# Later pairs' attention in eight groups, one TensorE burst per layer step

## The chip, the cores and the metric

The kernel runs on one core of one Trainium2 chip. The metric is device time in microseconds of one execution; lower is better.

## What is computed

Attention at two scales over four batches of eight heads (576 tokens, head width 64), then two feed-forward layers over the 2304 tokens of width 512, inner width 2048. All in fp32.

```python
# down-sampled: means over 4 tokens, softmax attention over 144, repeated 4 times
out_d = sm_attn(q_d, k_d, v_d)
out_up = np.repeat(out_d, 4, axis=2)
# local: only keys with |i - j| < 4
scores = np.where(mask, scale * q @ k.T, -1e9)
attn = softmax(scores)
x = out_up + attn @ v
...
h = x @ w_in;  g = np.maximum(0.01 * h, h);  x = g @ w_out      # layer 1
h = x @ w_in;  g = h - np.tanh(h);           out = g @ w_out    # layer 2
```

## The kernel before

Two heads make a *pair*; there are 16 pairs. Attention of one pair is cut into 17 *steps* (`STEPS`), and every engine has an `attention(step, ...)` that does its share: steps 0 to 3 turn q and k with the tensor engine (TensorE) and copy them out on ScalarE, step 4 computes the local scores, step 6 the down-sampled ones, steps 5 to 10 are the softmax (VectorE maximum, shift and sums; ScalarE exponentials; GpSimd the products with the inverse sums, `pl` at L993 and `pd` at L998), 11 to 14 turn the probabilities (L391, L396), 15 and 16 multiply by v. Two PSUM banks are shared by the steps and handed over by semaphores (`bank_full`, `bank_free`).

The first four pairs run alone (`batch0`). Then layer 1 runs in 8 tiles of 288 tokens. The first six (`MIXED`) are *mixed*: between their matmuls stand the steps of two later pairs each. Within a tile, f runs over the 16 blocks of the inner width (`CF`). At each f, TensorE does `hidden1(f)`, called H(f) below, 12 matmuls into the PSUM bank `ph1[f % 2]`, and `down1(f - 2)`, called D(f - 2), 12 matmuls into `acc`. Every product of fp32 numbers is split in a high part (rounded to fp32r) and a low part (the difference), three matmuls a product. Between H(f) and D stand these elementwise operations:

- ScalarE: `leak`, 0.01 h into `g1` (L684); VectorE: the maximum of leak and h (L887); ScalarE: the rounding `g_hi` (L664, in `split_g`); VectorE: `g_lo` (L872, in `lo_of_g1`).
- For f from 8 on, weights are split as they come: ScalarE `in_hi` (L648) and `out_hi` (L652), GpSimd `in_lo` (L1009) and `out_lo` (L1014).
- `next_x` (`ahead`) splits the next tile's x: `x_hi` (L657), `x_lo` (L867). The next tile's H(0) runs before D(15) of this one. `keep_y` copies the finished `acc` back.

The order is written out by hand, engine by engine. Slot 2f stands behind H(f) and slot 2f + 1 behind D(f - 2); a function `later` gives the step of a slot, four ahead (`HEAD`), since `batch0` has done the first four of pair 4's steps:

```python
def later(slot, tile):
    return (slot + HEAD) % STEPS, A, 2 * tile + 2 + (slot + HEAD) // STEPS
```

ScalarE rounds g_hi(f - 1) behind leak(f); `next_x` and `out_hi(15)` stand ahead of g_hi(15).

Of the kernel before, what the change touches and what calls it, by code (L numbers as in the profile page):

```python
# [24 lines left out]
ALU = mybir.AluOpType  # L25
# [14 lines left out]
HEAD = 4  # L40
KEPT_SLOTS = (20, 25)
# [16 lines left out]
def two_scale_attention_and_feed_forward(nc, q, k, v, w_in1, w_out1, w_in2, w_out2, out):  # L58
# [36 lines left out]
    with ExitStack() as ctx:  # L95
# [146 lines left out]
        def later(slot, tile):  # L242

            return (slot + HEAD) % STEPS, A, 2 * tile + 2 + (slot + HEAD) // STEPS
# [116 lines left out]
        def _(pe):  # L361
# [117 lines left out]
            def hidden1(tile, f):  # L479
# [7 lines left out]
                wait_from(pe, g_done, n - 1)  # L487
# [22 lines left out]
            def layer1(tile, between, begun=True, ahead=True):  # L510
                for f in range(CF + LAG1):
                    if f < CF and not (begun and f == 0):
                        hidden1(tile, f)
                    between(2 * f)
# [4 lines left out]
                    between(2 * f + 1)  # L519
# [44 lines left out]
            def mixed(tile, slots=2 * STEPS, begun=True):  # L564
                def between(slot):
                    if slot < slots:
                        attention(*later(slot, tile))
                layer1(tile, between, begun)

            def nothing(slot):  # L570
                pass

# [5 lines left out]
            mixed(0, begun=False)  # L578
            with pe.Fori(1, MIXED - 1) as tile:
                mixed(tile)  # L580
            mixed(MIXED - 1, 2 * STEPS - HEAD)
            for tile in range(MIXED, TILES1):
                layer1(tile, nothing, ahead=tile < TILES1 - 1)
# [7 lines left out]
        def _(act):  # L591
# [80 lines left out]
            def layer1(tile, between, extra, keep_before, ahead):  # L672
# [28 lines left out]
            def mixed(tile, keep_before, slots=2 * STEPS):  # L701
                def between(slot):
                    if slot < slots:
                        attention(*later(slot, tile))
                layer1(tile, between, nothing, keep_before, lambda: next_x(tile + 1))
# [94 lines left out]
        def _(dve):  # L800
# [79 lines left out]
            def layer1(tile, between, extra, keep_before, ahead):  # L880
                for f in range(CF + 1):
                    n = CF * tile + f
                    if f == CF:
                        ahead()
# [230 lines left out]
```

## Time and profile before

| | us |
|---|---|
| median of three runs | 989.72 |
| lowest and highest | 986.1, 992.62 |
| profiled execution, whole | 990.84 |
| its span | 989.1 |
| TensorE busy in it | 956.0 |
| mean granted TensorE clock | 0.984 |

The profile is of one execution on the one core. Times in its rows are from the span's start. In the rows, PE is TensorE's matmuls, PEld its weight loads, DVE VectorE, ACT ScalarE, POOL GpSimd, SP SyncE; PEclk is the granted share of the tensor clock, 1.00 being 2.4 GHz and 0.50 being 1.2 GHz.

### The profile page before, as it was taken

How to read it: one execution, taken by the hardware profiler on the slowest of the kernel's cores; microseconds unless marked ns; L12 is line 12 of the kernel's file. 1: busy time of each engine (PE TensorE's matmuls, PEld its weight loads, DVE VectorE, ACT ScalarE, POOL GpSimd, SP SyncE). 2: the span in 40 equal slices, each digit the busy share in tenths (PEclk: the TensorE clock that was granted, in tenths of full speed). 3: DMA queues.
4: the chain of work that ended last, by engine and by line, in shares of the span. 5: the costliest groups of instructions: out<-in, count | busy, mean ns of one | idle time of the engine just before them, and what ended most of it. 6: DMA issues, size and time to landing. Idle time of an engine off the chain costs nothing.

```text
span 989.1 us, 19759 instructions
## 1 busy us (share of the span) xinstructions
PE 956.0 (97%) x6960; PEld 892.1 (90%) x6960; DVE 579.4 (59%) x1066; ACT 554.5 (56%) x1355; POOL 411.5 (42%) x341
## 2 busy tenths in 40 slices
PE   6789999999999999999999999999999999999998
PEld 5678999999999999999999988889899899898996
DVE  5745653664556446635324766776676676766764
ACT  4445644544635446446354767775575666766654
POOL 4535732723616417227161837623233233233232
PEclk9769999999999999999999999999999999999999
DMA  7842421022112211210100302100000000000000
GB/s 168 179 138 66 112 50 35 16 49 49 25 24 49 49 25 24 49 27 10 55 1 30 110 24 76 42 33 1 1 32 1 32 0 0 32 0 0 32 1 32
DMA packets 87797, 41.48 MB, mean 42 GB/s; under 512 B 60352, under 2 KB 81344, under 8 KB 87744
## 3 DMA queue, kind: packets, MB, share of 16 engines
q1 hardware_dynamic: 87744, 40.78, 15.7%
q8 instruction: 33, 0.54, 0.2%
q14 instruction: 20, 0.16, 0.1%
HBM read 36.04 MB, written 4.72 MB: 41 GB/s over the span
## 4 chain that ended last, share of the span: by engine, by line
PE 78%; ACT 6%; DVE 6%; POOL 5%; issue 3%; DMA 2%; SPq 0%; ACTq 0%; POOLq 0%; DVEq 0%
PE ph L474 12%; PE ph L476 11%; PE ph L475 11%; PE acc L550 6%; PE acc L551 6%; PE acc L552 6%; PE acc L503 6%; PE acc L504 5%; PE acc L505 5%; PE banks L372 3%; PE banks L404 2%; DVE g_lo L872 2%; POOL pl L993 2%; PE banks L391 2%; POOL g_lo L1039 1%
## 5 line engine op out<-in xcount | busy, mean ns | idle before, releaser
L1039 POOL TENSOR_TENSOR g_lo<-scratch,g_hi 128x384 fp32r<-128x384 f32 x96 | 126.1, 1314 | 259.3 <-ACT g_hi L664 259.3
L887 DVE TENSOR_TENSOR g<-g,ph 128x288 f32<-128x288 f32 x128 | 57.9, 452 | 189.4 <-ACT g L684 188.5
L1009 POOL TENSOR_TENSOR in_lo<-w_whole,in_hi 128x512 fp32r<-128x512 f32 x64 | 83.8, 1310 | 160.9 <-ACT in_hi L648 159.7
L474 PE MATMUL ph<-x_hi,w_hi_a 128*128 128x288 f32 (+1 forms) x448 | 144.7, 323 | 1.9 <-DVE x_lo L867 1.9
L684 ACT ACTIVATE g<-ph 128x288 f32<-128x288 f32 x128 | 52.5, 410 | 157.2 <-PE ph L476 155.8
L476 PE MATMUL ph<-x_hi,w_lo_a 128*128 128x288 f32 (+1 forms) x448 | 140.5, 314 | 0.0
L475 PE MATMUL ph<-x_lo,w_hi_a 128*128 128x288 f32 (+1 forms) x448 | 140.4, 313 | 0.0
L923 DVE SCALAR_TENSOR_TENSOR scratch<-scratch,ph 128x384 f32<-128x384 f32 x96 | 53.2, 554 | 112.9 <-ACT scratch L729 108.0
L1014 POOL TENSOR_TENSOR out_lo<-w_whole,out_hi 128x512 fp32r<-128x512 f32 x64 | 86.4, 1350 | 56.3 <-ACT out_hi L652 55.6
L728 ACT ACTIVATE scratch<-ph 128x384 f32<-128x384 f32 x96 | 46.8, 488 | 108.4 <-PE ph L476 106.8
L872 DVE TENSOR_TENSOR g_lo<-g,g_hi 128x288 fp32r<-128x288 f32 x128 | 88.6, 692 | 2.7 <-ACT g_hi L664 2.7
L474 PEld LDWEIGHTS ph<-x_hi,w_hi_a 128*128 128x128 f32 x448 | 84.9, 189 | 5.2 <-issue 3.1
L475 PEld LDWEIGHTS ph<-x_lo,w_hi_a 128*128 128x128 f32 x448 | 84.9, 190 | 1.4
L476 PEld LDWEIGHTS ph<-x_hi,w_lo_a 128*128 128x128 f32 x448 | 84.9, 189 | 0.0
L503 PE MATMUL acc<-g_hi,out_hi 128*128 128x288 f32 x256 | 79.1, 309 | 2.5 <-DVE g_lo L872 2.5
L503 PE MATMUL acc<-g_hi,w_hi_a 128*128 128x288 f32 x256 | 78.7, 307 | 1.9 <-DVE g_lo L872 1.9
L474 PE MATMUL ph<-x_hi,in_hi 128*128 128x288 f32 x256 | 78.8, 308 | 0.0
L504 PE MATMUL acc<-g_lo,w_hi_a 128*128 128x288 f32 x256 | 76.0, 297 | 0.0
L505 PE MATMUL acc<-g_hi,w_lo_a 128*128 128x288 f32 x256 | 75.9, 296 | 0.0
L505 PE MATMUL acc<-g_hi,out_lo 128*128 128x288 f32 x256 | 75.6, 295 | 0.0
L475 PE MATMUL ph<-x_lo,in_hi 128*128 128x288 f32 x256 | 75.6, 295 | 0.0
L504 PE MATMUL acc<-g_lo,out_hi 128*128 128x288 f32 x256 | 75.5, 295 | 0.0
(162 smaller groups left out, 2688.8 us busy)
## 6 DMA issues: line engine op xcount, KB each, us to landing
out_dram<-o_stage SPq DMA_DIRECT2D x18, 256.0 KB, 2.0
w_whole<-in_moe_w_in_dram SPq DMA_DIRECT2D x16, 256.0 KB, 3.6
w_whole<-in_moe_w_out_dram SPq DMA_DIRECT2D x16, 256.0 KB, 4.4
qn<-in_q_dram SPq DMA_DIRECT2D x28, 144.0 KB
kn<-in_k_dram SPq DMA_DIRECT2D x28, 144.0 KB
v4n<-in_v_dram SPq DMA_DIRECT2D x28, 144.0 KB
vw<-in_v_dram SPq DMA_DIRECT2D x28, 122.5 KB
scratch<-in_moe_w_in_dram SPq DMA_DIRECT2D x8, 256.0 KB, 2.9
```

The source lines that it names most:

```text
L474: pe.matmul(bank, whi, x_hi[:, c, 0:width], start=(c == 0), stop=False)
L475: pe.matmul(bank, whi, x_lo[:, c, 0:width], start=False, stop=False)
L476: last = pe.matmul(bank, wlo, x_hi[:, c, 0:width], start=False, stop=(c == CD - 1))
L503: pe.matmul(acc[:, c, 0:T1], whi, g1_hi[:, f % 3, :], start=(f == 0), stop=False)
L504: pe.matmul(acc[:, c, 0:T1], whi, g1_lo[:, f % 3, :], start=False, stop=False)
L505: last = pe.matmul(acc[:, c, 0:T1], wlo, g1_hi[:, f % 3, :], start=False, stop=(f == CF - 1))
L550: pe.matmul(acc[:, j, 0:DM], hi, whi, start=(f == 0), stop=False)
L551: pe.matmul(acc[:, j, 0:DM], hi, wlo, start=False, stop=False)
L872: dve.tensor_tensor(g1_lo[:, f % 3, :], g1[:, f % 2, :], g1_hi[:, f % 3, :].bitcast(F32), ALU.subtract).then_inc(g_lo_done, 1)
L1009: pool.tensor_tensor(in_lo[:, f % 2, :], w_whole[:, f - KEPT, 0:DM], in_hi[:, f % 2, :].bitcast(F32), ALU.subtract).then_inc(in_lo_done, 1)
L1014: pool.tensor_tensor(out_lo[:, f % 2, :], w_whole[:, f - KEPT, DM:CW], out_hi[:, f % 2, :].bitcast(F32), ALU.subtract).then_inc(out_lo_don ...
L1039: pool.tensor_tensor(g2_lo[:, f % 3, :], g2[:, f % 2, :], g2_hi[:, f % 3, :].bitcast(F32), ALU.subtract).then_inc(g_lo_done, 1)
```

## The change

The steps are taken in eight groups (`GROUPS`), one group at each f, and all of TensorE's part of a group runs as one burst behind D(f - 2). The last two f of a tile take groups 0 and 1 of the pair after (`GROUP_HEAD`). VectorE's local maximum and shift move from step 6 into step 5 and so stand in the scores' group. The maximum is written into the PSUM bank in place, and g_hi and g_lo read it there; so ScalarE rounds g_hi(f) at the same f as its leak, and H(f) waits for `g_lo_done` of f - 2, not `g_done`. `next_x` stands at f = 15 right behind g_hi(15) and g_lo(15). `split_in(f + 2)` stands right behind leak(f), and `split_out(f)` at the end of f.

```diff
+GROUPS = ((0, 1), (2, 3), (4, 5), (6, 7, 8), (9, 10), (11, 12), (13, 14), (15, 16))
+GROUP_HEAD = 2
-        def later(slot, tile):
-            return (slot + HEAD) % STEPS, A, 2 * tile + 2 + (slot + HEAD) // STEPS
+        def later(f, tile, last):
+            if f < last:
+                pair, group = divmod(f + GROUP_HEAD, len(GROUPS))
+                for step in GROUPS[group]:
+                    yield step, A, 2 * tile + 2 + pair
...
 # TensorE, hidden1
-                wait_from(pe, g_done, n - 1)
+                wait_from(pe, g_lo_done, n - 1)
...
 # TensorE, layer1
                     if f < CF and not (begun and f == 0):
                         hidden1(tile, f)
-                    between(2 * f)
                     if ahead and f == CF + LAG1 - 1:
                         hidden1(tile + 1, 0)
                     if f >= LAG1:
                         down1(tile, f - LAG1)
-                    between(2 * f + 1)
+                    for step, s, i in later(f, tile, last):
+                        attention(step, s, i)
...
 # ScalarE, layer1
-                    if f == CF:
-                        ahead()
-                    if f - 1 >= KEPT:
-                        split_out(tile, f - 1)
                     if f < CF:
                         act.wait_ge(h_done, n + 1)
-                        wait_from(act, g_lo_done, n - 1)
+                        wait_from(act, g_done, n - 1)
                         act.activation(g1[:, f % 2, :], ph1[:, f % 2, 0:T1], ACT.Copy, scale=0.01)\
                             .then_inc(leak_done, 1)
                     if f == 0:
                         keep_before()
-                    if f:
-                        split_g(n - 1, f - 1, g1[:, (f - 1) % 2, :], g1_hi)
-                    between(2 * f)
                     if KEPT <= f + 2 < CF:
                         split_in(tile, f + 2)
+                    if f < CF:
+                        split_g(n, f, ph1[:, f % 2, 0:T1], g1_hi)
+                    if f == CF - 1:
+                        ahead()
+                    for step, s, i in later(f, tile, last):
+                        attention(step, s, i)
                     extra(f)
-                    between(2 * f + 1)
+                    if KEPT <= f < CF:
+                        split_out(tile, f)
...
 # VectorE
-                elif step == 6:
                     dve.wait_ge(s.bank_free[1], uses1(i, 3))
                     dve.tensor_reduce(s.mxl[:, :], s.pl[:, :, :], AX_X, ALU.max).then_inc(s.max_l, 1)
...
-                dve.tensor_tensor(g1_lo[:, f % 3, :], g1[:, f % 2, :], g1_hi[:, f % 3, :].bitcast(F32),
+                dve.tensor_tensor(g1_lo[:, f % 3, :], ph1[:, f % 2, 0:T1], g1_hi[:, f % 3, :].bitcast(F32),
                                   ALU.subtract).then_inc(g_lo_done, 1)
...
-                        dve.tensor_tensor(g1[:, f % 2, :], g1[:, f % 2, :], ph1[:, f % 2, 0:T1], ALU.max)\
+                        dve.tensor_tensor(ph1[:, f % 2, 0:T1], g1[:, f % 2, :], ph1[:, f % 2, 0:T1], ALU.max)\
                             .then_inc(g_done, 1)
...
 # GpSimd, layer1
-                    if f - 1 >= KEPT:
-                        split_out(tile, f - 1)
-                    between(2 * f)
                     if KEPT <= f + 2 < CF:
                         split_in(tile, f + 2)
-                    between(2 * f + 1)
+                    for step, s, i in later(f, tile, last):
+                        attention(step, s, i)
+                    if KEPT <= f:
+                        split_out(tile, f)
```

What this makes of the order is shown at two places, both in the second pair of a mixed tile, f = 9 to 11. On ScalarE, before, from leak(9) on (L684 leak, L664 g_hi, L648 in_hi, L652 out_hi, L607 the local exponential, L611 the down-sampled ones, L616 a copy of turned probabilities):

```order
301 L684 ACTIVATE g<-ph 128x288
302 L664 ACTIVATE g_hi<-g 128x288
303 L648 ACTIVATE in_hi<-w_whole 128x512
304 L652 ACTIVATE out_hi<-w_whole 128x512
305 L684 ACTIVATE g<-ph 128x288
306 L664 ACTIVATE g_hi<-g 128x288
307 L607 ACTIVATE pl<-pl 128x630
308 L648 ACTIVATE in_hi<-w_whole 128x512
309 L611 ACTIVATE pd,rs<-banks,mxd 96x144 x3
310 L652 ACTIVATE out_hi<-w_whole 128x512
311 L684 ACTIVATE g<-ph 128x288
```

and after, from leak(9) on (L676 leak, L660 g_hi, L644 in_hi, L648 out_hi, L603 and L607 the exponentials):

```order
302 L676 ACTIVATE g<-ph 128x288
303 L644 ACTIVATE in_hi<-w_whole 128x512
304 L660 ACTIVATE g_hi<-ph 128x288
305 L603 ACTIVATE pl<-pl 128x630
306 L607 ACTIVATE pd,rs<-banks,mxd 96x144 x3
307 L648 ACTIVATE out_hi<-w_whole 128x512
308 L676 ACTIVATE g<-ph 128x288
309 L644 ACTIVATE in_hi<-w_whole 128x512
310 L660 ACTIVATE g_hi<-ph 128x288
```

The exponentials stood at f = 10 around in_hi(12); now they stand at f = 9, ahead of out_hi(9), and leak(10) and in_hi(12) come behind them.

On GpSimd, before, at the same place (L986 the value sums `vd`, L1009 in_lo, L1014 out_lo, L993 the norm of the local probabilities, L998 that of the down-sampled ones):

```order
110 L1014 TENSOR_TENSOR out_lo<-w_whole,out_hi 128x512
111 L1009 TENSOR_TENSOR in_lo<-w_whole,in_hi 128x512
112 L1014 TENSOR_TENSOR out_lo<-w_whole,out_hi 128x512
113 L993 TENSOR_TENSOR pl<-pl,rs 128x630
114 L1009 TENSOR_TENSOR in_lo<-w_whole,in_hi 128x512
115 L998 TENSOR_TENSOR pd<-pd,rs 96x432
116 L1014 TENSOR_TENSOR out_lo<-w_whole,out_hi 128x512
```

and after (L997 in_lo, L1002 out_lo, L981 and L986 the norms):

```order
108 L997 TENSOR_TENSOR in_lo<-w_whole,in_hi 128x512
109 L1002 TENSOR_TENSOR out_lo<-w_whole,out_hi 128x512
110 L997 TENSOR_TENSOR in_lo<-w_whole,in_hi 128x512
111 L981 TENSOR_TENSOR pl<-pl,rs 128x630
112 L986 TENSOR_TENSOR pd<-pd,rs 96x432
113 L1002 TENSOR_TENSOR out_lo<-w_whole,out_hi 128x512
114 L997 TENSOR_TENSOR in_lo<-w_whole,in_hi 128x512
```

The local norm came behind out_lo(10) and ahead of in_lo(13); now it comes one block earlier, behind in_lo(12).

On TensorE the local probabilities were turned in two bursts of four with D(10) between them, the first behind H(12). Now they are turned in one burst behind D(9) (L508 to L510 down1, L396 the turning, L479 and L480 hidden1):

```order
1217 L508 MATMUL acc<-g_hi,out_hi 128x288
1218 L509 MATMUL acc<-g_lo,out_hi 128x288
1219 L510 MATMUL acc<-g_hi,out_lo 128x288
1220 L396 MATMUL banks<-ident,pl 70x128 x8
1221 L479 MATMUL ph<-x_hi,in_hi 128x288
1222 L480 MATMUL ph<-x_lo,in_hi 128x288
```

where before stood

```order
1242 L475 MATMUL ph<-x_lo,in_hi 128x288
1243 L476 MATMUL ph<-x_hi,in_lo 128x288
1244 L391 MATMUL banks<-ident,pl 70x128 x4
1245 L503 MATMUL acc<-g_hi,out_hi 128x288
1246 L504 MATMUL acc<-g_lo,out_hi 128x288
```

## Rows read from the trace of the kernel before

**Rows 1.** The page: busy time of TensorE, its share of the span, matmuls

```profile
PE 956.0 (97%) x6960; PEld 892.1 (90%) x6960; DVE 579.4 (59%) x1066; ACT 554.5 (56%) x1355; POOL 411.5 (42%) x341
```

**Rows 2.** Two stages: length, busy of PE, PEld, DVE, ACT, POOL, then PEclk, DMA

```profile
272.20:339.80 67.60, 66.75 (x618) 64.12 (x618) 35.97 (x70) 33.44 (x89) 29.76 (x27) 1.00 0.16 36
...
468.50:577.00 108.50, 107.42 (x803) 106.60 (x802) 52.64 (x90) 56.41 (x124) 46.84 (x33) 1.00 0.15 47
```

**Rows 3.** Waits of TensorE from 137 to 577 us, all there are

```profile
PE banks L391 <- POOL pl L993: 2.7, 10, 0.3
PE acc L503 <- DVE g_lo L872: 2.5, 7, 0.8
```

**Rows 4.** Timeline of TensorE around a burst: start, duration, operation

```profile
300.52 0.38 PE L503 MATMUL acc<-g_hi,w_hi_a 128*128 128x288 f32 x1
300.74 0.29 PE L504 MATMUL acc<-g_lo,w_hi_a 128*128 128x288 f32 x1
```

**Rows 5.** Timeline of TensorE at the entry into a values burst

```profile
262.94 0.29 PE L505 MATMUL acc<-g_hi,out_lo 128*128 128x288 f32 x1
263.16 1.15 PE L404 MATMUL banks<-pT,vw 70*64 70x64 f32 x32
```

**Rows 6.** Timeline of TensorE at its waits; recorded idle time in brackets

```profile
79.12 0.40 PE L503 MATMUL acc<-g_hi,w_hi_a 128*128 128x288 f32 x1 [1.91 <-DVE g_lo L872]
...
272.29 0.40 PE L503 MATMUL acc<-g_hi,out_hi 128*128 128x288 f32 x1 [0.26 <-DVE g_lo L872]
...
284.38 0.29 PE L505 MATMUL acc<-g_hi,w_lo_a 128*128 128x288 f32 x1
285.00 0.63 PE L391 MATMUL banks<-ident,pl 128*70 128x128 f32 x4 [0.32 <-POOL pl L993]
...
320.10 0.62 PE L391 MATMUL banks<-ident,pl 128*70 128x128 f32 x4 [0.26 <-POOL pl L993]
...
575.87 0.37 PE L503 MATMUL acc<-g_hi,out_hi 128*128 128x288 f32 x1 [0.77 <-DVE g_lo L872]
```

**Rows 7.** Timeline of ScalarE: the first down-sampled exponential and out_hi behind the third

```profile
315.47 0.38 ACT L611 ACTIVATE pd<-banks,mxd 96x144 f32<-96x144 f32 x1
...
316.55 0.63 ACT L652 ACTIVATE out_hi<-w_whole 128x512 fp32r<-128x512 f32 x1
```

**Rows 8.** Timeline of VectorE: a shift alone, then the second pair's work beside GpSimd

```profile
279.63 0.81 DVE L834 TENSOR_TENSOR pl<-pl,mxl 128x630 f32<-128x630 f32 x1
...
307.79 0.52 DVE L823 TENSOR_TENSOR pl<-banks,band 128x350 f32<-128x350 f32 x1 [0.82 <-PE banks L372]
308.23 0.74 DVE L824 TENSOR_REDUCE kdT<-kT 128x144 f32<-128x576 f32 x1
...
311.51 0.81 DVE L832 TENSOR_REDUCE mxl<-pl 128x9 f32<-128x630 f32 x1
312.35 1.83 DVE L834 TENSOR_TENSOR pl<-pl,mxl 128x630 f32<-128x630 f32 x1
...
317.50 0.46 DVE L887 TENSOR_TENSOR g<-g,ph 128x288 f32<-128x288 f32 x1 [0.39 <-ACT g L684]
317.88 0.99 DVE L872 TENSOR_TENSOR g_lo<-g,g_hi 128x288 fp32r<-128x288 f32 x1
```

**Rows 9.** Timeline of GpSimd around the second pair's norm, and one norm alone

```profile
283.62 1.24 POOL L993 TENSOR_TENSOR pl<-pl,rs 128x630 f32<-128x630 f32 x1 [9.18 <-DVE rs L849]
...
312.22 1.29 POOL L1014 TENSOR_TENSOR out_lo<-w_whole,out_hi 128x512 fp32r<-128x512 f32 x1
...
317.26 1.30 POOL L1014 TENSOR_TENSOR out_lo<-w_whole,out_hi 128x512 fp32r<-128x512 f32 x1 [0.42 <-ACT out_hi L652]
318.51 1.46 POOL L993 TENSOR_TENSOR pl<-pl,rs 128x630 f32<-128x630 f32 x1
```

**Rows 10.** Busy time and granted clock around the stop in tile 0

```profile
77.00:79.00 2.00, 0.21 (x2) 0.00 (x0) 2.00 (x3) 1.94 (x7) 1.76 (x1) 1.00 0.60 132
...
79.65:83.07 3.42, 3.42 (x17) 3.32 (x16) 2.12 (x7) 0.47 (x2) 2.75 (x2) 0.50 0.01 1
```

More of the change, by code:

```diff
@@ L506, in down1, with layer1 @@
                 last.then_inc(y_done, 1)
-            def layer1(tile, between, begun=True, ahead=True):
+            def layer1(tile, last, begun=True, ahead=True):
                 for f in range(CF + LAG1):
@@ L562, in layer2 @@
                         down2(tile, f - LAG2)
[L564 to L571, printed above, removed]
             pe.wait_ge(const_ready, 1)
@@ L699, in next_x, with mixed @@
                 split_x(x1_hi, T1, tile, CF * tile)
[L701 to L705, printed above, removed]
+            def mixed(tile, keep_before, last=CF):
+                layer1(tile, last, nothing, keep_before, lambda: next_x(tile + 1))
             def nothing(f=None):
@@ L780, in _ @@
                 mixed(tile, lambda: keep_y(tile - 1))
-            mixed(MIXED - 1, lambda: keep_y(MIXED - 2), 2 * STEPS - HEAD)
+            mixed(MIXED - 1, lambda: keep_y(MIXED - 2), CF - GROUP_HEAD)
             for tile in range(MIXED, TILES1):
                 last = tile == TILES1 - 1
-                layer1(tile, nothing, w2a if last else nothing, lambda: keep_y(tile - 1),
+                layer1(tile, 0, w2a if last else nothing, lambda: keep_y(tile - 1),
                        nothing if last else lambda: next_x(tile + 1))
@@ L890, in layer1, with mixed @@
                         keep_before()
-                    if f:
-                        lo_of_g1(n - 1, f - 1)
-                    between(2 * f)
+                    if f < CF:
+                        lo_of_g1(n, f)
+                    if f == CF - 1:
+                        ahead()
+                    for step, s, i in later(f, tile, last):
+                        attention(step, s, i, (i + 2) // CD, (i + 2) % CD)
                     extra(f)
-                    between(2 * f + 1)
             def next_x(tile):
                 lo_of_x(x1_hi, x1_lo, T1, tile, CD * tile)
-            def mixed(tile, keep_before, slots=2 * STEPS):
-                def between(slot):
-                    if slot < slots:
-                        step, s, i = later(slot, tile)
-                        attention(step, s, i, (i + 2) // CD, (i + 2) % CD)
-                layer1(tile, between, nothing, keep_before, lambda: next_x(tile + 1))
+            def mixed(tile, keep_before, last=CF):
+                layer1(tile, last, nothing, keep_before, lambda: next_x(tile + 1))
             def nothing(f=None):
@@ L958, in _ @@
                 mixed(tile, lambda: keep_y(tile - 1))
-            mixed(MIXED - 1, lambda: keep_y(MIXED - 2), 2 * STEPS - HEAD)
+            mixed(MIXED - 1, lambda: keep_y(MIXED - 2), CF - GROUP_HEAD)
             for tile in range(MIXED, TILES1):
                 last = tile == TILES1 - 1
-                layer1(tile, nothing, w2a if last else nothing, lambda: keep_y(tile - 1),
+                layer1(tile, 0, w2a if last else nothing, lambda: keep_y(tile - 1),
                        nothing if last else lambda: next_x(tile + 1))
@@ L1015, in split_out, with layer1 @@
                                    ALU.subtract).then_inc(out_lo_done, 1)
-            def layer1(tile, between):
-                for f in range(CF + 1):
+            def layer1(tile, last):
+                for f in range(CF):
                     if isinstance(tile, int) and tile == 0 and EARLY <= f + 2 < KEPT:
                         split_kept(f + 2)
-                    if f - 1 >= KEPT:
-                        split_out(tile, f - 1)
-                    between(2 * f)
                     if KEPT <= f + 2 < CF:
                         split_in(tile, f + 2)
-                    between(2 * f + 1)
-            def mixed(tile, slots=2 * STEPS):
-                def between(slot):
-                    if slot < slots:
-                        attention(*later(slot, tile))
-                layer1(tile, between)
-            def nothing(slot):
-                pass
+                    for step, s, i in later(f, tile, last):
+                        attention(step, s, i)
+                    if KEPT <= f:
+                        split_out(tile, f)
             def lo_of_g2(tile, f):
```

22 lines of the change are left out of this document (10 added, 12 removed).

## The prediction

> **What bounds the kernel now.** I read the page first: TensorE is busy for 956.0 of 989.1 us [rows 1], so only what stops TensorE, or what it does beyond its arithmetic, can be gained. The table by stage [rows 2] then says where. The first stage (pairs 0 to 3, 64 us) keeps its order: groups 0 and 1 of the later pairs are the same four steps that it already does, and between VectorE's steps 5 and 6 it has nothing else to do. Layer 1 without attention (108.5 us) is 107.42 us busy, nothing to win. The steady mixed tile takes 67.6 us and is 66.75 us busy, and there are six mixed tiles; the change lives there. The chain of waits of TensorE over 137 to 577 us holds only two kinds [rows 3]: ten waits for the normalised local probabilities (transposes, L391, on GpSimd's L993) and seven for g_lo (L503 on VectorE's L872), 5.2 us together as recorded.
>
> The recorded idle time understates a stop, since a matmul's end is modelled: it is recorded 0.29 us long, yet the next starts 0.13 us after it. At 284.38 the last matmul of a product starts, at 285.00 the transposes: 0.62 less the normal 0.13 is 0.49 us lost, where 0.32 is recorded as idle [rows 6]. So a stop costs its recorded idle plus 0.16 or 0.17.
>
> **Terms of a steady mixed tile, what goes.** A "product" is the 12 matmuls of hidden1 or down1: 12 x 0.133 = 1.6 us.
>
> (a) Joints. After an attention burst the first matmul of a product needs 0.22 us until the next starts, not 0.13: 300.52 to 300.74, behind a burst of four transposes [rows 4]. That is 0.09 us for each return to the products. Going in costs nothing before transposes but 0.09 before scores and values: 262.94 to 263.16 [rows 5]. Before, one tile has 23 bursts (12 steps with TensorE work in each of two pairs, one meeting the next pair's). After, seven groups of each pair have TensorE work: 14 bursts. 9 x 0.09 = 0.81. Of the entries into scores or values 6 become 4: 0.18. Together -0.99 us. The matmuls themselves stay.
>
> (b) Waits that are there now: at the tile's start 0.26 + 0.17 = 0.43 for g_lo(15), in the first pair 0.49, in the second 0.26 + 0.16 = 0.42 [rows 6]. The first goes: the rounding g_hi(15), which stood behind next x and out_hi, now comes right after max(15). The second goes: TensorE still has five products between scores and transposes, but VectorE takes max and shift right behind the scores' additions; followed through with the durations used below, the norm lands some 9.5 us after the scores start, and TensorE comes at 10.4. So -1.34 us, before what replaces the third.
>
> **What is late next.** I follow the second pair of a tile; times are from the start of its scores, T. Scores take 1.62 and step 6 0.64 us until the next product starts, a first product after a burst 1.69. TensorE: scores to 1.62, H(9) 3.31, D(7) 4.90, step 6 5.54, H(10) 7.22, D(8) 8.82, H(11) 10.42, D(9) 12.0. There the eight transposes stand now; before, H(12) came first and they were due at 13.6. The price of one burst per layer step is one product less of cover here.
>
> VectorE: the first addition starts at 1.72 as now (307.79, the scores having started at 306.07), kd 0.44 later and 0.74 long, the second addition like the first, max 3.3 to 4.1 (0.81), shift from 4.14 [rows 8]. The shift takes 0.81 us at 279.63 but 1.83 at 312.35 [rows 8], where GpSimd had started a 1.28 us subtraction at 312.22 [rows 9]: it ran 0.67 us after that ended. GpSimd does in_lo(10), the three vd additions and out_lo(8) back to back until 4.43, so the shift ends at 5.1. Then max(9) of the leak to 5.5 and, new, ScalarE waits for it: g_hi(9) to 5.98, lo(9) 6.02 to 6.47, the maximum of the down-sampled scores to 7.0. ScalarE's three exponentials with their reads occupy 1.08 us (315.47 to 316.55) [rows 7]: 7.0 to 8.1. Only behind them stands out_hi(9), 0.63: 8.73. GpSimd: out_lo(9) 8.78 to 10.06, just before D(9) asks for it at 10.42. leak(10) and in_hi(12) stand behind out_hi(9) on ScalarE: 9.56, and in_lo(12) stands in front of the norm on GpSimd: 10.06 to 11.34. The norm itself 1.25 to 1.46 [rows 9]: 12.75. The transposes wait from 12.0 to 12.8: +0.78 us where 0.42 was. in_lo(13), out_lo(10) and out_lo(11) behind it have 0.3 to 1.5 us to spare: D(10) starts 3.3 us after the wait ends, out_lo(10) needs 1.1 (step 10) + 1.28.
>
> In that chain lo(9) is free of GpSimd because it now reads a PSUM bank. The row for it: at 317.50 the maximum L887 (one operand in PSUM) takes 0.46 us while out_lo runs from 317.26, and L872 at 317.88 (both operands in SBUF) 0.99, ending 0.31 after out_lo [rows 8, 9]. I take the first as lo's price, 0.45; the other end is 1.0 to 1.3, a rival below. The Trainium skill ("SBUF — State Buffer", section "SBUF: two separate sides") says that a VectorE op "with two SBUF inputs" is locked out by a GpSimd op that reads SBUF for the whole instruction, and by that the PSUM operand takes lo out of the lock; the trace agrees on L887, and for lo itself no run here shows it. That rule gives the sum above, its absence the rival's.
>
> Tile boundary: H(15) ends at 0, x_hi (four roundings, 1.43) 1.47 to 2.8, the k copies to 3.6, out_hi(15) to 4.1, out_lo(15) to 5.43; D(15) is due at 5.35: +0.1. x_lo ends at 3.6, H of the next tile is due at 3.75. Step 6 of the first pair needs kd, done 0.2 us before. The new wait of hidden1 for g_lo in place of g_done costs nothing while lo(f) is done 2.6 us after H(f) and H(f+2) comes after 6.4; queued behind it would be the whole product.
>
> A steady tile: -0.99 - 1.34 + 0.78 + 0.10 = **-1.45 us**; tiles 1 to 4, **-5.8**.
>
> **The other tiles.** Tile 0 also splits the kept weights. There TensorE stood 1.9 us before 79.12 [rows 6] and then ran 3.4 us at half clock [rows 10]. After, I get w_lo(4) ending at 79.8 and the norm at 81.0, with TensorE there at 78.65: a wait of 2.4 us in place of 1.9 and 1.0, the same slow stretch, at H(5) +0.3. Rest of the tile: joints -0.9, waits 0.34 and 0.51 gone, 0.88 new. Tile 0: -0.6. Tile 5 (attention ends at f = 13): -0.81 joints, -0.49 and -0.34 waits, +0.78, boundary -0.1: -0.9. Tile 7's last product waits 0.77 + 0.16 for g_lo(15) [rows 6]; then only out_lo(15) is left, 0.5: -0.4. The operations on VectorE, ScalarE and GpSimd are the same in number; TensorE is the bound, so a change of 0.1 us in them is bounded by the chain above. DMA issues on SyncE wait for the same attention steps; k and v of the next pair are needed some 20 us later.
>
> **Sum:** -5.8 - 0.6 - 0.9 - 0.4 = -7.7 us. The profiled execution took 990.84 us (span 989.1), so 983.1; the median of the three runs lies 1.1 lower, 989.72, so **982.0 us**, -0.8%.
>
> **Rivals.**
> A, no new wait: step 8's chain is shorter than I hold (the shift meets no GpSimd op, the exponentials begin 0.8 us earlier). Then 6 x 0.78 + 5 x 0.10 = 5.2 us more: 976.8. For: the shift at 279.63 took 0.81. Against: at T + 4.1 GpSimd always has vd or out_lo in hand, and out_hi, in_lo and norm are in series.
> B, lo still takes turns with GpSimd: lo(9) and lo(10) end 0.3 to 0.9 later, out_lo(9) lands at 10.6 (D(9) waits 0.2) and the norm at 13.6 (wait 1.3). 1.53 in place of 0.78, six times: +4.5, 986.5.
> C, slower: the wait before the transposes grows to the size of the one in tile 0, and the clock falls with it. The granted clock went to 0.50 (1.2 GHz) for 3.42 us after TensorE stood 1.9 us [rows 10, 6], and not after the 0.77 us at 575.87 (clock 1.00 over that stage [rows 2]). At half clock a matmul takes 0.24 us, so 3.42 us do the work of 1.9: 1.5 us lost. With a wait of 2.4: 6 x (1.6 + 1.5) = 18.6 over the forecast, 1000.6. It decides from a wait of that size, 1.9 us, that is, the norm at T + 13.9. For: six operations in series on three engines stand before it. Against: it needs 1.1 us more than my chain.
> D, nothing moves: joints saved in one place are paid in more waits elsewhere in the tiles (k and q copies, values), 987 to 994. The order shows that the bursts do merge, so that half is no guess.
>
> **Chances.** Forecast (979 to 985.5) 0.45, A 0.2, B 0.17, C 0.08, D 0.10. One per cent, about what a measurement of this kernel tells from no change, is 9.9 us: faster than 979.8 are A and a small part of the forecast's own spread, 0.27; slower than 999.6 is C, 0.07; the rest 0.66. The range takes A's and B's ends and D's middle and leaves out C: 975 to 993.
>
> **What the profile after would show.** 14 bursts in a tile, tile length 66.1 us; no g_lo wait at a tile's start; the wait of the transposes on the norm gone in each first pair and 0.6 us idle as recorded (0.8 in full) in each second; lo at 0.45 beside GpSimd; tile 0 with one stop of 2 to 2.5 us and about 3.4 us at half clock. I would be wrong first in the second pair: if the exponentials start before T + 6.2 the wait is gone, if after T + 8.2 it is rival C.

## The result, and the profile after

The changed kernel takes 982.33 us (median of 6 runs, 979.99 to 984.38) where the kernel before takes 988.95 (6 runs, 986.1 to 992.62). The ratio is 0.9922, with a 95% interval of 0.9898 to 0.9945: 0.8% faster, within the 1% that I had called no change, but the interval lies clear of 1, so the gain is real. The profiled execution took 982.79 us, its span is 981.0.

The page's engine line, and the group of g_lo in its fifth part, which stood at 88.6 us, mean 692 ns, before:

```profile
PE 951.6 (97%) x6960; PEld 893.9 (91%) x6960; DVE 552.4 (56%) x1066; ACT 560.1 (57%) x1355; POOL 406.8 (41%) x341
...
L864 DVE TENSOR_TENSOR g_lo<-ph,g_hi 128x288 fp32r<-128x288 f32 x128 | 58.6, 458 | 59.1 <-ACT g_hi L660 59.1
```

TensorE is still busy 97% of the span; VectorE has 27 us less to do than in [rows 1]. g_lo's group alone gives back 30; the records of an engine overlap a little, so groups don't sum to its busy time.

The windows of the steady mixed tile and of the stage without attention, columns as in [rows 2]:

```profile
272.37:338.42 66.05, 65.65 (x619) 64.01 (x619) 32.38 (x68) 34.03 (x88) 29.20 (x27) 1.00 0.16 37
462.50:571.20 108.70, 108.02 (x807) 107.15 (x806) 48.39 (x90) 58.24 (x123) 46.21 (x34) 1.00 0.13 39
```

The tile went from scores to scores in 67.57 us before (274.10 to 341.67) and now takes 66.05. From tile 0's first scores to the start of layer 2 it was 510.25 us and is 501.79: 8.46 less. The first stage, which the change doesn't touch, took 2.2 us more in this execution and layer 2 1.8 less, and the span is 8.1 shorter.

The waits of TensorE between 130 and 571 us, columns as in [rows 3] (the view leaves out idle times too short to count, such as the 0.05 us at a tile boundary):

```profile
PE banks L396 <- POOL pl L981: 1.7, 5, 0.4
PE acc L508 <- POOL out_lo L1002: 0.5, 1, 0.5
```

No wait for g_lo is left, and five waits for the norm where there were ten: one in each second pair. TensorE's timeline at the stop in tile 0, then in the first and in the second pair of the fourth tile:

```profile
80.35 0.29 PE L510 MATMUL acc<-g_hi,w_lo_a 128*128 128x288 f32 x1
83.14 1.07 PE L396 MATMUL banks<-ident,pl 128*70 128x128 f32 x8 [2.50 <-POOL pl L981]
...
282.65 0.30 PE L510 MATMUL acc<-g_hi,w_lo_a 128*128 128x288 f32 x1
282.78 1.04 PE L396 MATMUL banks<-ident,pl 128*70 128x128 f32 x8
...
315.25 0.29 PE L510 MATMUL acc<-g_hi,out_lo 128*128 128x288 f32 x1
315.90 1.06 PE L396 MATMUL banks<-ident,pl 128*70 128x128 f32 x8 [0.36 <-POOL pl L981]
```

In the first pair the transposes start 0.13 us behind the last matmul of down1, at full pace. In the second they start 0.65 behind it: 0.52 us lost. In tile 0 it is 2.65.

The chain that leads to that 0.52 starts with the second pair's scores at T = 303.36. VectorE's part of it:

```profile
306.65 0.81 DVE L824 TENSOR_REDUCE mxl<-pl 128x9 f32<-128x630 f32 x1
307.50 0.88 DVE L826 TENSOR_TENSOR pl<-pl,mxl 128x630 f32<-128x630 f32 x1
308.30 0.45 DVE L877 TENSOR_TENSOR ph<-g,ph 128x288 f32<-128x288 f32 x1
309.23 0.46 DVE L864 TENSOR_TENSOR g_lo<-ph,g_hi 128x288 fp32r<-128x288 f32 x1 [0.48 <-ACT g_hi L660]
...
313.21 0.46 DVE L864 TENSOR_TENSOR g_lo<-ph,g_hi 128x288 fp32r<-128x288 f32 x1 [0.48 <-ACT g_hi L660]
313.58 1.01 DVE L845 TENSOR_SCALAR rs<-rs 96x3 f32<-96x3 f32 x1
```

ScalarE's, the first down-sampled exponential and out_hi(9):

```profile
310.23 0.38 ACT L607 ACTIVATE pd<-banks,mxd 96x144 f32<-96x144 f32 x1 [0.42 <-DVE mxd L832]
...
311.31 0.62 ACT L648 ACTIVATE out_hi<-w_whole 128x512 fp32r<-128x512 f32 x1
```

And GpSimd's, which holds three operations in a row, the last of them the norm:

```profile
306.41 1.29 POOL L1002 TENSOR_TENSOR out_lo<-w_whole,out_hi 128x512 fp32r<-128x512 f32 x1
...
312.02 1.29 POOL L1002 TENSOR_TENSOR out_lo<-w_whole,out_hi 128x512 fp32r<-128x512 f32 x1 [2.50 <-ACT out_hi L648]
313.27 1.29 POOL L997 TENSOR_TENSOR in_lo<-w_whole,in_hi 128x512 fp32r<-128x512 f32 x1
314.52 1.25 POOL L981 TENSOR_TENSOR pl<-pl,rs 128x630 f32<-128x630 f32 x1
```

The norm's inputs were there long before: the reciprocal L841 ran at 311.16, 3.4 us before the norm started. The norm stood in GpSimd's queue behind out_lo(9) and in_lo(12). out_lo(9) waits for out_hi(9), which stands behind the exponentials on ScalarE, and in_hi(12) comes behind out_hi(9). The norm ends at T + 12.4.

### The profile page after: what moved, and what is told of

Read it like the earlier page. It is cut to its first block, busy times and chain, and to the rows that moved or that the text cites. A ratio compares the mean times of both kernels' runs of the same rounds, so it can differ in the third digit from the quotient of the medians.

```text
span 981.0 us, 19759 instructions
## 1 busy us (share of the span) xinstructions
PE 951.6 (97%) x6960; PEld 893.9 (91%) x6960; DVE 552.4 (56%) x1066; ACT 560.1 (57%) x1355; POOL 406.8 (41%) x341
## 4 chain that ended last, share of the span: by engine, by line
PE 83%; POOL 6%; ACT 4%; DVE 3%; issue 3%; DMA 1%; ACTq 0%; POOLq 0%; DVEq 0%
PE ph L479 13%; PE ph L481 12%; PE ph L480 12%; PE acc L555 6%; PE acc L556 6%; PE acc L557 6%; PE acc L508 6%; PE acc L509 6%; PE acc L510 6%; PE banks L377 3%; PE banks L409 2%; PE banks L396 2%; PE banks L370 2%; POOL in_lo L997 1%; POOL pl L981 1%
## 5 line engine op out<-in xcount | busy, mean ns | idle before, releaser
L877 DVE TENSOR_TENSOR ph<-g,ph 128x288 f32<-128x288 f32 x128 | 58.9, 460 | 166.8 <-ACT g L676 166.5
L479 PE MATMUL ph<-x_hi,w_hi_a 128*128 128x288 f32 (+1 forms) x448 | 144.4, 322 | 2.1 <-DVE x_lo L859 1.9
L997 POOL TENSOR_TENSOR in_lo<-w_whole,in_hi 128x512 fp32r<-128x512 f32 x64 | 84.5, 1320 | 144.2 <-ACT in_hi L644 143.6
L480 PE MATMUL ph<-x_lo,w_hi_a 128*128 128x288 f32 (+1 forms) x448 | 140.9, 315 | 0.0
L676 ACT ACTIVATE g<-ph 128x288 f32<-128x288 f32 x128 | 52.5, 410 | 138.1 <-PE ph L481 138.0
L1002 POOL TENSOR_TENSOR out_lo<-w_whole,out_hi 128x512 fp32r<-128x512 f32 x64 | 85.9, 1343 | 72.5 <-ACT out_hi L648 72.3
L864 DVE TENSOR_TENSOR g_lo<-ph,g_hi 128x288 fp32r<-128x288 f32 x128 | 58.6, 458 | 59.1 <-ACT g_hi L660 59.1
L479 PEld LDWEIGHTS ph<-x_hi,w_hi_a 128*128 128x128 f32 x448 | 85.1, 190 | 5.0 <-issue 2.7
L480 PEld LDWEIGHTS ph<-x_lo,w_hi_a 128*128 128x128 f32 x448 | 85.1, 190 | 1.4
L660 ACT ACTIVATE g_hi<-ph 128x288 fp32r<-128x288 f32 x128 | 52.7, 411 | 47.4 <-DVE ph L877 46.8
L479 PE MATMUL ph<-x_hi,in_hi 128*128 128x288 f32 x256 | 79.1, 309 | 0.0
L508 PE MATMUL acc<-g_hi,out_hi 128*128 128x288 f32 x256 | 76.9, 300 | 0.7 <-POOL out_lo L1002 0.5
L508 PE MATMUL acc<-g_hi,w_hi_a 128*128 128x288 f32 x256 | 75.9, 296 | 0.0
L510 PE MATMUL acc<-g_hi,out_lo 128*128 128x288 f32 x256 | 75.9, 296 | 0.0
L510 PE MATMUL acc<-g_hi,w_lo_a 128*128 128x288 f32 x256 | 75.8, 296 | 0.0
```

What stands on the lines that cost most here:

```text
L479: pe.matmul(bank, whi, x_hi[:, c, 0:width], start=(c == 0), stop=False)
L480: pe.matmul(bank, whi, x_lo[:, c, 0:width], start=False, stop=False)
L508: pe.matmul(acc[:, c, 0:T1], whi, g1_hi[:, f % 3, :], start=(f == 0), stop=False)
L510: last = pe.matmul(acc[:, c, 0:T1], wlo, g1_hi[:, f % 3, :], start=False, stop=(f == CF - 1))
L877: dve.tensor_tensor(ph1[:, f % 2, 0:T1], g1[:, f % 2, :], ph1[:, f % 2, 0:T1], ALU.max)\
L997: pool.tensor_tensor(in_lo[:, f % 2, :], w_whole[:, f - KEPT, 0:DM], in_hi[:, f % 2, :].bitcast(F32), ALU.subtract).then_inc(in_lo_done, 1)
```

## The experiments

Each edit is against the changed kernel, but for the last two, which start from the kernel before. "The tile" is scores to scores of the same mixed tile (the fourth), 66.05 us in the changed kernel and 67.57 before. All kernels of one series ran beside the kernel before on the same chip: its medians there are 992.26 (first four), 991.15 (next four) and 991.71 (last two). The changed kernel's 982.33 was measured beside a median of 988.95, so compare the ratios with its 0.9922 and not the times: beside 992.26 that ratio is 984.5 us. No experiment moved the weights' splits alone (`split_in` ahead of g_hi, `split_out` at the end of f); their part of the gain was not separated.

### Two bursts in a layer step, and half of the steps in each

```diff
+SECOND = (1, 3, 12, 14, 16)
                     if f < CF and not (begun and f == 0):
                         hidden1(tile, f)
+                    if 0 < f <= CF:
+                        for step, s, i in later(f - 1, tile, last):
+                            if step in SECOND:
+                                attention(step, s, i)
...
-                    for step, s, i in later(f, tile, last):
-                        attention(step, s, i)
+                    if f < CF:
+                        for step, s, i in later(f, tile, last):
+                            if step not in SECOND:
+                                attention(step, s, i)
```

> The changed kernel, but TensorE takes the second step of a group (steps 1, 3, 12, 14, 16) behind the next hidden product instead of in the same burst; the other engines keep the order of the change. Theory 1 (joints cost 0.09 us each): 10 more joints in a mixed tile and two more entries into the values, 0.2 us: +1.1 us on the tile's 66.05, so 67.1 to 67.2, and some 6 us in all (988). Rival (only waits were won, a joint costs nothing since the weight load hides it): tile 66.0 to 66.2, time as the changed kernel's 982.

Measured: 993.34 us (10 runs), ratio to before 1.0016 (0.9988 to 1.0044); the tile takes 68.06. The first pair, which has no wait in either kernel, went from 30.99 to 31.46: +0.47, the joints alone. Five returns at 0.09 are 0.45 of it. For a tile's two pairs that makes 0.94. The tile came out 0.9 us over what was expected, and the rest of the +2.0 is waits that came with the split: the norm now costs 0.82 us in the second pair, and the pieces that stand behind the next hidden1 hold up the copies and out_lo:

```profile
PE acc L509 <- POOL out_lo L1009: 3.5, 11, 0.5
PE banks L397 <- POOL pl L988: 3.2, 5, 0.7
```

So the joints are as costly as I said, and a joint more also delays what is queued behind it: with two bursts the whole gain is gone.

### The old slots, with the rest of the change

```diff
+        def at_slot(slot, tile, last):
+
+            if slot < (2 * STEPS if last == CF else 2 * STEPS - 4) and last:
+                yield (slot + 4) % STEPS, A, 2 * tile + 2 + (slot + 4) // STEPS
...
 # TensorE
+                    for step, s, i in at_slot(2 * f, tile, last):
+                        attention(step, s, i)
                     if ahead and f == CF + LAG1 - 1:
                         hidden1(tile + 1, 0)
                     if f >= LAG1:
                         down1(tile, f - LAG1)
-                    for step, s, i in later(f, tile, last):
+                    for step, s, i in at_slot(2 * f + 1, tile, last):
                         attention(step, s, i)
```

On the other three engines both slots' steps stand together where the group stood, so this isn't the order of the kernel before there.

> The changed kernel with the old 34 slots for the attention steps on all engines; the early rounding from PSUM, next x behind the last rounding and the shift in step 5 stay. Theory 1: joints 0.99 us back, the transposes' wait on the norm (0.52 us in the second pair) gone since hidden(12) covers it again: tile 66.5, time about 985. If merging is where nearly all came from: tile 67.0 or more, 988. If the early rounding and the earlier shift were all of it: 66.05 or less, 982 or less.

Measured: 1000.21 us (10 runs), ratio 1.0089 (1.0058 to 1.0119); the tile takes 69.59, three us more than expected. The expectation missed: the rest of the change without the groups is slower than the kernel before. Its waits between 200 and 480 us:

```profile
PE banks L401 <- POOL pl L990: 7.3, 7, 1.7
PE banks L375 <- ACT qT L598: 3.7, 4, 0.9
```

Of the tile's +3.5, a wait of 1.69 recorded stands before the transposes of the second pair (the norm starts only at 321.26, behind out_lo and in_lo), and at the boundary the k and q turns wait for ScalarE's copies, which now stand behind the four roundings of next x. The groups are thus no mere saving of joints. They also place the steps where the new order of the layer's work leaves room. How much of the +3.5 is the old slots and how much their place on the other engines was not separated.

### g back in SBUF

```diff
-                        wait_from(act, g_done, n - 1)
+                        wait_from(act, g_lo_done, n - 1)
...
-                        split_g(n, f, ph1[:, f % 2, 0:T1], g1_hi)
+                        split_g(n, f, g1[:, f % 2, :], g1_hi)
...
-                dve.tensor_tensor(g1_lo[:, f % 3, :], ph1[:, f % 2, 0:T1], g1_hi[:, f % 3, :].bitcast(F32),
+                dve.tensor_tensor(g1_lo[:, f % 3, :], g1[:, f % 2, :], g1_hi[:, f % 3, :].bitcast(F32),
...
-                        dve.tensor_tensor(ph1[:, f % 2, 0:T1], g1[:, f % 2, :], ph1[:, f % 2, 0:T1], ALU.max)\
+                        dve.tensor_tensor(g1[:, f % 2, :], g1[:, f % 2, :], ph1[:, f % 2, 0:T1], ALU.max)\
```

> The changed kernel, but the maximum is written to the SBUF buffer and read there by both roundings as before, so that g_lo has two SBUF operands; order and TensorE's waits are those of the change. Theory (g_lo takes turns with GpSimd when both operands lie in SBUF): g_lo 0.8 to 1.3 us where it meets in_lo or out_lo, norm of the second pair later, transposes wait 1.2 to 1.5 us instead of 0.5: tile 66.8, in all +4 us (986). Rival (the place of g does not matter): g_lo slower but the tile 66.05.

Measured: 987.96 us (10 runs), ratio 0.9958 (0.9931 to 0.9986); the tile takes 66.71, and its window shows where it comes from:

```profile
274.50:341.21 66.71, 65.68 (x619) 64.04 (x619) 37.61 (x68) 34.45 (x88) 30.29 (x27) 1.00 0.16 36
```

VectorE is busy for 37.61 us instead of 32.38 with the same 68 instructions, and the transposes' wait in the second pair grew from 0.36 to 0.96 recorded. This is rival B's world, and its size (+0.75 a tile) is nearly right: +0.66. The way there is another. g_lo(9) takes 0.58 us, only 0.12 more than in the changed kernel, the shift 1.09 instead of 0.88, and the exponentials start 0.37 later, at T + 7.24. The other 0.29 us is lost on GpSimd, whose in_lo(12) takes 1.58 us instead of 1.29 beside a g_lo that keeps its 0.46:

```profile
315.74 0.46 DVE L864 TENSOR_TENSOR g_lo<-g,g_hi 128x288 fp32r<-128x288 f32 x1 [0.51 <-ACT g_hi L660]
315.77 1.58 POOL L997 TENSOR_TENSOR in_lo<-w_whole,in_hi 128x512 fp32r<-128x512 f32 x1
```

So the operation that started first kept its pace here, and the other paid.

### The shift back in step 6

```diff
                     dve.tensor_tensor(s.pl[:, NBA:NB, :], src, band[:, NBA:NB, :], ALU.add).then_inc(s.bank_free[1], 1)
+                elif step == 6:
                     dve.wait_ge(s.bank_free[1], uses1(i, 3))
```

> The changed kernel with VectorE's local maximum and shift back in step 6, that is in the group one layer step later, behind maximum(9) and g_lo(9). Theory (a chain of exponentials, out_hi, out_lo, in_lo, norm stands behind the shift): exponentials about 1 us later, wait of the transposes in the second pair 1.5 us instead of 0.52, in the first 0 to 0.3: tile 67.1, in all +6 us (988). If other things bound the norm: tile 66.05 to 66.3.

Measured: 985.95 us (8 runs), ratio 0.9927 (0.9895 to 0.9959), which doesn't tell it from the changed kernel; the tile does, at 66.83 (+0.78, expected +1.05). The transposes' wait is 0.83 us in full in the second pair (0.67 recorded), and D(9) ahead of them starts 0.28 late, behind an out_lo(9) that ends 0.06 before it. In the first pair the transposes start some 0.03 us late. The exponentials came 0.7 us later, at T + 7.57, where about 1 was expected.

### Next x at f = 16

```diff
+                    if f == CF:
+                        ahead()
...
-                    if f == CF - 1:
-                        ahead()
```

on ScalarE and VectorE.

> The changed kernel with next x one place later, behind the last group of attention and out_hi(15). Theory: x_hi ends at 5.0 instead of 2.8 us after hidden(15), the next tile's first product is due 3.75 us after it and gets its first x_lo at 4.7: +0.95 us for a mixed tile's boundary, 0.15 for an unmixed one: tile 67.0, in all +5 us (987). Rival (x was in time anyway, the g_lo(15) in front was the whole of the old wait): tile 66.05.

Measured: 999.59 us (5 runs), ratio 1.0093 (1.0062 to 1.0125); the tile takes 68.67, +2.6 where 0.95 was expected. VectorE at the boundary:

```profile
337.91 3.90 DVE L859 TENSOR_TENSOR x_lo<-xT,x_hi 128x288 fp32r<-128x288 f32 x4 [0.36 <-ACT x_hi L653]
```

and GpSimd beside it:

```profile
337.50 1.27 POOL L1002 TENSOR_TENSOR out_lo<-w_whole,out_hi 128x512 fp32r<-128x512 f32 x1 [2.49 <-ACT out_hi L648]
338.75 0.94 POOL L974 TENSOR_TENSOR vd<-v4n 72x256 f32<-72x256 f32 x1
339.76 1.74 POOL L974 TENSOR_TENSOR vd<-vd,v4n 72x256 f32<-72x256 f32 x2
```

In the changed kernel the same four x_lo take 1.56 us, from 333.13, while GpSimd rests. One layer step later they meet out_lo(15) and the value sums and take turns with them one by one. TensorE, which takes x_lo a quarter at a time, waits for each of the four quarters (1.13, 0.24, 0.25 and 0.25 recorded). My expectation counted the place of x_lo in the queue and not what runs beside it.

### The norm ahead of in_lo

```diff
                 for f in range(CF):
+                    for step, s, i in later(f, tile, last):
+                        if step == 9:
+                            attention(step, s, i)
                     if isinstance(tile, int) and tile == 0 and EARLY <= f + 2 < KEPT:
                         split_kept(f + 2)
                     if KEPT <= f + 2 < CF:
                         split_in(tile, f + 2)
                     for step, s, i in later(f, tile, last):
-                        attention(step, s, i)
+                        if step != 9:
+                            attention(step, s, i)
```

> The changed kernel, but GpSimd does the local norm (step 9) ahead of in_lo(f + 2) and of the kept weights' split. Theory (the norm is ready to start in the second pair when out_lo(9) ends, and stands one 1.28 us subtraction behind it for no reason): no wait of the transposes in the second pair, 0.5 us less a tile (65.55); in tile 0 the stop of 2.65 us ahead of the transposes becomes a wait of about 1 us for the kept weights, and the clock stays at 1.00: 3 us less there; in all -5 to -6 us (976.5). Rival: in_lo(12) is then late for hidden(12) and takes the gain back: tile 66.05. Rival on the clock: it falls in tile 0 even so.

Measured: 977.43 us (6 runs), ratio 0.9867 (0.9836 to 0.9898); the tile takes 65.70. The view of waits shows none for TensorE between 137 and 480 us; the 0.2 us at each tile boundary (0.04 recorded) stays. GpSimd's timeline:

```profile
305.71 1.30 POOL L1002 TENSOR_TENSOR out_lo<-w_whole,out_hi 128x512 fp32r<-128x512 f32 x1 [2.50 <-ACT out_hi L648]
306.97 1.25 POOL L981 TENSOR_TENSOR pl<-pl,rs 128x630 f32<-128x630 f32 x1
308.17 1.29 POOL L997 TENSOR_TENSOR in_lo<-w_whole,in_hi 128x512 fp32r<-128x512 f32 x1
```

The norm ends at 308.22, and TensorE comes for it 0.9 us later:

```profile
308.95 0.29 PE L510 MATMUL acc<-g_hi,out_lo 128*128 128x288 f32 x1
309.08 0.38 PE L396 MATMUL banks<-ident,pl 128*70 128x128 f32 x2
```

In tile 0 the norm comes ahead of the kept weights' low part, and the 2.50 recorded becomes 0.96 before hidden1 (L479, for `w_lo_a`). No slow stretch follows it. Tile 0 is 2.5 us shorter (68.30 against 70.78), but not all of it is the norm's place. 1.6 is the shorter stop, and 1.5 the slow stretch that is missing. Against that, the half clock from the first stage lasts longer here (to 69.21, that is 2.9 us into the tile and not 1.4) and takes 0.7 back. Whether the shorter stop kept the clock up one execution can't say: in the next experiment it stayed up behind a stop of 2.23. Tiles 1 to 4 are 0.35 shorter each, 1.4 together.

### keep_y behind g_lo(0)

```diff
 # ScalarE
-                    if f == 0:
-                        keep_before()
...
                         split_g(n, f, ph1[:, f % 2, 0:T1], g1_hi)
+                    if f == 0:
+                        keep_before()
...
 # VectorE
+                    if f < CF:
+                        lo_of_g1(n, f)
                     if f == 0:
                         keep_before()
-                    if f < CF:
-                        lo_of_g1(n, f)
```

> The changed kernel with the copy of the finished sum (keep_y) behind g_hi(0) and g_lo(0) on ScalarE and VectorE. Theory: hidden(2) of an unmixed tile no longer waits 0.31 us for g_lo(0), two tiles: -0.6 us; in mixed tiles nothing waits there, so nothing there; 981.7. Rival: down(0) then waits for the copy: mixed tile longer than 66.05.

Measured: 981.72 us (6 runs), ratio 0.9899 (0.9869 to 0.9929); the tile takes 66.09. In the tiles without attention the two products H(1) and H(2) take 3.17 us, as before the change, and not 3.51. In the changed kernel VectorE had there

```profile
468.05 0.46 DVE L877 TENSOR_TENSOR ph<-g,ph 128x288 f32<-128x288 f32 x1 [1.92 <-ACT g L676]
469.36 0.82 DVE L870 COPY xT<-acc 128x288 f32<-128x288 f32 x2 [0.85 <-PE acc L510]
470.40 0.46 DVE L864 TENSOR_TENSOR g_lo<-ph,g_hi 128x288 fp32r<-128x288 f32 x1 [0.22 <-ACT g_hi L660]
```

so g_lo(0) stood behind two copies that wait for the last product of the tile before, and H(2), which now needs the bank that g_lo(0) reads, started at 471.00 and not at 470.74. From tile 0's first scores to layer 2 this execution took 499.64 us, 2.1 less than the changed kernel's. Only 0.6 of it is the edit, as expected. The other 1.5 lies in tile 0, where the edit changes nothing (`keep_before` is `nothing` there): the clock didn't fall behind the stop in this execution.

### Both of these

Both edits together.

> Both of the last two together: the sum of both, -6 us against the changed kernel: 976.

Measured: 977.33 us (7 runs), ratio 0.9864 (0.9841 to 0.9888); the tile takes 65.71. It is the fastest of all, but not to be told from the norm's move alone.

### The early rounding in the old order

From the kernel before: the maximum in PSUM, g_hi(f) and g_lo(f) at f, with the waits that this needs, nothing else. ScalarE's part of the edit:

```diff
-                    if f:
-                        split_g(n - 1, f - 1, g1[:, (f - 1) % 2, :], g1_hi)
+                    if f < CF:
+                        split_g(n, f, ph1[:, f % 2, 0:T1], g1_hi)
```

> The kernel before with one part of the change: maximum in PSUM, g_hi(f) and g_lo(f) at the same f, hidden(f) waiting for g_lo(f - 2). Slots, next x, shift in step 6 as before. Theory: the 0.43 us wait for g_lo(15) at a tile's start goes, the transposes' two waits (0.49 and 0.42) and the joints stay: tile 67.1 instead of 67.57, in all -2.5 us against before. Rival (the new order of ScalarE delays in_hi and the copies as in old_slots): tile 68 or more.

Measured: 1000.72 us (4 runs), ratio 1.0092 (1.006 to 1.0125); the tile takes 68.77, 1.2 us more than before, where less was expected. Its waits from 130 to 580 us:

```profile
PE banks L391 <- POOL pl L993: 9.3, 10, 1.5
PE acc L503 <- POOL out_lo L1014: 1.4, 4, 0.4
```

The wait for g_lo is gone, and the norm's came to 9.3 us from 2.7 [rows 3]. Why, VectorE's timeline in the first pair shows:

```profile
285.93 0.46 DVE L887 TENSOR_TENSOR ph<-g,ph 128x288 f32<-128x288 f32 x1 [0.58 <-ACT g L684]
286.87 0.46 DVE L872 TENSOR_TENSOR g_lo<-ph,g_hi 128x288 fp32r<-128x288 f32 x1 [0.48 <-ACT g_hi L664]
287.25 0.80 DVE L845 TENSOR_REDUCE rs<-pl 128x9 f32<-128x630 f32 x1
```

The sum L845, whose exponential was under way from 284.87, stands behind g_lo, and g_lo behind ScalarE's g_hi, which stands behind the maximum L887. Rounding at the same f makes the two engines wait for each other in turn, about half a microsecond at each handover (0.58 and 0.48 above), and whatever is queued behind waits too.

### The same, with the shift in step 5

> The same with the local maximum and shift in step 5 as well, old slots and old place of next x. Theory: both of the transposes' waits go too, since the norm comes 0.7 to 0.9 us earlier and ScalarE and GpSimd keep out_hi, in_hi and the norm in their old order: tile 66.2 to 66.4, -7 us against before; the merging of bursts (0.99 us a tile) less its new wait (0.52) is then what the change adds. Rival: the tile stays at 67.1 or over, and the shift only pays within the grouped order.

The edit is the one above, and the line `elif step == 6:` ahead of the maximum taken out.

Measured: 988.99 us (10 runs), ratio 0.9971 (0.9947 to 0.9995); the tile takes 67.48 where 66.2 to 66.4 was expected. Waits of 0.34 and 0.59 us before the transposes remain. So from before to after the tile goes 67.57, +1.20 (early rounding) to 68.77, -1.29 (shift) to 67.48, -1.43 (groups, next x and the new places of the splits, together) to 66.05. Of the last, 0.9 is the joints; how the rest divides was not tried. The parts don't add up in another order: the shift is worth 0.78 with groups and 1.29 without.

## Why the prediction was right

**The sum.** From tile 0's first scores to layer 2 the change gave back 8.46 us, forecast 7.7; the median fell to 982.33, forecast 982.0. The before median of the same comparison lies 0.8 under that of the first three runs, so the gain in medians is 6.6, and part of that match is luck: the first stage's length varies more than the terms do (below). Tile 0 has a piece of luck too: the half clock that both executions bring along from the first stage ends 2.1 us after the first scores before and 1.4 after, worth 0.34 of the 8.46.

**(a) Joints**, -0.99 a tile. Shown: +0.47 a pair without any wait in the two-burst kernel. In the changed kernel itself the tile's -1.52 is -1.33 of waits gone (0.48, 0.43 and 0.42 by the same starts as in [rows 6]), +0.52 and +0.21 of waits come, and -0.92 left for the joints.

**(b) Waits that go**, -1.34. As forecast all three went, but for the first pair the reason was told too simply. I credited the shift's place. Moving the shift pays for the early rounding, which costs 1.2 by itself; 0.34 us of wait remained in that pair until the groups came as well.

**The new wait**, forecast 0.78, measured 0.52. The chain came in nearly step by step: shift at T + 4.14 as forecast, its end at T + 5.0 (5.1), the exponentials at T + 6.87 (7.0), out_hi(9) at T + 7.95 (8.1), the norm's end at T + 12.4 (12.75). In that execution the shift took 0.88 us and 0.07 of it at most was a turn for GpSimd, which I had put at 0.15. The mechanism was right. The term was 0.26 too large because the links came 0.1 to 0.35 us early. The norm's move takes the whole wait away though the exponentials stay where they were. The shift back in step 6 lengthens it by starting them later. So both ends of the chain set the wait, and what I had called the price of one burst (a product less of cover) could be saved by one operation's place.

**g_lo free of GpSimd** [rows 8, 9]: at 313.21 it takes 0.46 us while out_lo and in_lo run (312.02 to 314.5). With both operands in SBUF, VectorE's work in the tile grows by 5.2 us and the tile by 0.66, of which 0.29 is GpSimd's own in_lo(12) held up. The rule of the Trainium skill ("SBUF — State Buffer", section "SBUF: two separate sides"), that a VectorE operation with two SBUF inputs is shut out while a GpSimd operation that reads SBUF holds the ports, is borne out by that pair of kernels, and by next x at f = 16: 3.90 us for four against 1.56.

**Tile boundary**, forecast +0.10, measured +0.21 (0.05 of it recorded as idle): D(15) starts at 336.65 behind an out_lo(15) that ran from 335.23 for 1.29. The mechanism was right.

**Tile 0**, forecast -0.6 with a stop of 2.4 us and the same slow stretch: -0.94 (71.72 to 70.78), a stop of 2.65 and 3.4 us at a clock of 0.51. From H(2) on, behind the half clock of the first stage, it is -0.61 (66.82 to 66.21), so the forecast was right and 0.34 of the -0.94 luck. In the kernel with keep_y moved the clock didn't fall there and the tile took 69.26: 1.52 less, the 1.5 that rival C priced it at. The stop ends at the same place in both, 13.7 us after the first scores, and all of the 1.5 comes behind it. **Tile 5**, forecast -0.9: -1.2. **The end of layer 1**, -0.4: -0.33 (5.89 to 5.56).

**The step that failed** is one that the sum hardly felt: "the new wait of hidden1 for g_lo in place of g_done costs nothing". In tiles 6 and 7, where no attention stretches the steps, H(1) and H(2) follow each other and g_lo(0) stands behind keep_y: +0.34 each, gone (3.17 us for the two products again) when keep_y is moved. I had looked at the spacing within a tile, where H(f + 2) comes late, and not at the boundary, where three products of hidden1 come with one down1 between them. And one gain was not in the sum: in tile 7 VectorE also splits layer 2's weights, g_lo took turns with GpSimd there (1.18 us at 563.84 before, 0.46 now), and the products from H(12) to D(11) took 0.7 us longer than theirs do now. That tile ran 0.4 faster, 51.54 against 51.93 (from the end of one H(15) to the next), in spite of the +0.34. That g_lo's price is the cause there was not tried by itself.

**The rivals.** A needed the exponentials 0.8 us earlier: they came at T + 6.87. B is what g in SBUF would have been. C's slow stretches in every tile needed stops of the size of 1.9 us, and there were none but tile 0's. D did not happen.

## What to carry to other kernels

When one engine is busy for 97% of the span and yet the time moves with the order of work, write out the chain behind each of its stops and look at the in-order queue it passes last: here one operation moved ahead of another on an engine that is busy for 41% gave 4.2 us more between the first scores and layer 2, 3.4 of it without what the clock did in tile 0, where the change had given 7 to 8. A VectorE subtraction that runs beside GpSimd should have an operand in PSUM, or its place should be where GpSimd rests. Moving an elementwise step next to its producer puts a handover into two queues; it pays only if nothing urgent is queued behind it.

## What the runs showed of the hardware

The granted clock doesn't follow the length of a stop alone. In tile 0 it fell to half (1.2 GHz) after 1.91 us idle before the change and 2.50 after it, and after 3.05 with g in SBUF and 2.86 with the shift in step 6. It stayed at 1.00 after 2.23 with keep_y moved, 2.33 in the early-rounding kernel and 2.83 with two bursts. With next x at f = 16 it fell at 134.7 us behind four short stops (1.23, 0.18, 0.24 and 0.24), and the next scores came 1.4 us later than at the other boundaries. The changed kernel and the one with keep_y moved have the same order in tile 0, so this pair differs by the execution, not by the edit (columns of the windows as in [rows 2]; first the changed kernel):

```profile
84.50:87.90 3.40, 3.40 (x16) 3.40 (x16) 0.46 (x1) 1.96 (x4) 3.40 (x2) 0.51 0.00 0
```

and the kernel with keep_y moved:

```profile
83.00:88.00 5.00, 4.83 (x40) 4.81 (x41) 1.35 (x3) 3.02 (x7) 5.00 (x4) 1.00 0.00 0
```

What else decides it was not tried. A price from one execution that has such a stretch, like tile 0's with the norm moved, should be read with its 1.5 us taken out.

Much of the spread between executions lies in the first stage, where TensorE often waits for its inputs: in the twelve profiles tile 0's first scores start between 63.4 and 70.1 us, while layer 2 takes 407.4 to 409.6. The changed kernel's profile has 6.8, 6.8 and 17.1 us at half clock there (from 26.5, 43.6 and 53.8 us), that of the last version 17.1 and 6.8 (from 39.1 and 63.0), and tile 0's first H starts at 66.30 and 61.46 though the stage's order is the same. For a change of under 1% the time between two marks of the trace behind that stage says more than the total.

A very short operation on VectorE pays for GpSimd too: L845, three elements a partition, took 1.01 us at 313.58 and ended 0.03 after the in_lo that ran beside it. With GpSimd at rest it took 0.15 at 282.01 in the same kernel (and 0.10 in the early-rounding kernel, L853 at 288.42).
